# Turning each unit of the Fourier stage by identity products on the four quarters of the TensorE array

## The chip, the cores and the metric

The kernel runs on one core of a Trainium2 chip. The metric is the device time of one execution in microseconds (us). The kernel before was timed three times; the number used is the median. Engines are named as in the profile: PE is TensorE's matmul side, PEld its weight loads, DVE is VectorE, ACT is ScalarE, POOL is GpSimd, SP is SyncE, which here only issues transfers.

## The reference

```python
def reference(x, filt_r, filt_i, moe_w_in, moe_w_out, moe2_w_in, moe2_w_out):
    X = np.fft.rfft(x, axis=1)                     # x: (2, 3008, 256)
    y = np.fft.irfft(X * (filt_r + 1j * filt_i)[None], n=3008, axis=1)
    x = y.reshape(6016, 256).astype(np.float32)
    h = x @ moe_w_in                               # (256, 2048)
    x = np.maximum(0.01 * h, h) @ moe_w_out        # (2048, 256)
    h = x @ moe2_w_in
    r = np.maximum(h, 0.0)
    return (r * r) @ moe2_w_out
```

A filter along the sequence by Fourier transforms, and then two layers of matrix products, everything in float32.

## The kernel before, in words

The sequence length 3008 is 64 times 47, and the transform is done as one over 64 points and one over 47. The channels are worked on in two halves of 128. The first stage is `over_n1` (L906): products of the input with a table over the 64 points, whose results ACT and DVE copy out of PSUM into the tiles TT1A and TT1B, one for each half of the channels, with channels on the 128 partitions. Then come 16 units, eight for each half (UNITS, L15); a unit is four frequencies j (UJ = 4) of both batch rows. The tiles hold for each frequency a real and an imaginary part, each in a stretch of 64 columns of which 48 (R) hold data; the 16 columns between a real and an imaginary part are set to zero at the start (L347, semaphore `n1_pad`).

A unit i goes through these steps, each with its own banks of PSUM:

- `turn(i)` on PE (L922 to L939): eight full transposes, one for each batch row b and frequency k, each of a 128 x 112 piece of TT1 against the 128 x 128 identity `DM[:, 2, :]`. Batch row b goes to PSUM bank b. The last transpose of each batch row increments `s2_ps`.
- `turned(i)` on ACT (L526): two copies, one for each batch row, from bank b into the tile S2 (shown as S in the profile), each started by its own count of `s2_ps`; each increments `s2_sb`. S2 has two buffers.
- `spectrum(i)` on PE (L941): four products with the table TW over the 47 points, each 48 partitions x 64 columns with 512 moving columns (two of them are split in two for the first unit of a half). Real and imaginary rows and the two pairs of frequencies take different quarters of the array. It waits for both copies (`s2_sb` at 2i+2), writes banks 2 and 3 or 4 and 5 in turns, and increments `p_ps`.
- `filtered(i)` on DVE (L748): three operations from PSUM with the filter tile FL (L762, L766 twice), into AF and BF.
- two operations on POOL (L449, L450), which finish the complex product and increment `yf_sb`. Between units POOL also does some of the preparation of the first layer's weights (L351 to L369).
- `inverse(i)` on PE (L960): four products as in `spectrum`, out of AF, into banks 6 and 7. It waits for `yf_sb` and for the copies of the unit before.
- `back(i)` on ACT (L531): two copies from banks 6 and 7 into U.
- `store_u(i)` (L235): SP stores U to the DRAM tensor zu; when a half is complete `load_v` (L251) reads it back in another order as V.

`sequence(c)` (L980) does the last products of the transform out of V, and from L1019 on the two layers run; there each product is a sum of three passes (`passes`, `up`).

The order on PE is written out (L1001 to L1018). After a short start the loop over i issues `spectrum(i+2)`, `turn(i+3)`, `inverse(i)`. The last iterations carry four `sequence` steps of the first half between them (`drained`). The order on ACT (L600 to L614) is `turned(i+3)`, `back(i)`. So the copies of a turn stand between that turn and the next `spectrum` on PE, and `inverse` is what PE has to do meanwhile:

```python
for i in range(UNITS):
    if i + 2 < UNITS:
        spectrum(i + 2)
    if i + 3 < UNITS:
        turn(i + 3)
    if i >= UNITS - 3:
        for c in drained(i):
            sequence(c)
    inverse(i)
```

Ahead of everything PE does eight products of a zero tile WARM (L902) into bank 0.

A float32 product appears in the trace as two MATMUL records and two LDWEIGHTS records, a transpose as one of each.

Of the kernel before, what the change touches and what calls it, by code (L numbers as in the profile page):

```python
# [5 lines left out]
B, S, D, F = 2, 3008, 256, 2048  # L6
# [3 lines left out]
R = 2 * MH  # L10
IM = 64
KR = IM + R
UJ = 4
# [16 lines left out]
def fft_mlp_kernel(nc, x, filt, dft, tab, sgn, w1i, w1o, w2i, w2o, out):  # L30
    f32, f32r = mybir.dt.float32, mybir.dt.float32r
    ALU = mybir.AluOpType
    ACT = mybir.ActivationFunctionType
# [5 lines left out]
    def at(name, shape, dt, offset):  # L39
        return nc.alloc_sbuf_tensor_at(name, shape, dt, offset=base + offset)  # L40
# [13 lines left out]
    S2 = at("S2", [KR, 2, B, UJ, 128], f32, o_wo + 24 * KB)  # L54
    TT1A = at("TT1A", [128, B, 2 * NJ, IM], f32, o_x + 32 * KB)
    TT1B = at("TT1B", [128, B, 2 * NJ, IM], f32, o_x)
    TT1 = [TT1A, TT1B]
    DM = at("DM", [128, 3, 128], f32, o_s + 2 * KB)
# [27 lines left out]
    WARM = at("WARM", [128, 128], f32, o_s)  # L86
# [5 lines left out]
    with ExitStack() as ctx:  # L92
        def sem(name):
            return ctx.enter_context(nc.semaphore(name))

        PS = ctx.enter_context(nc.psum_tensor("PS", [128, 8, 512], f32))
# [11 lines left out]
        s2_ps = sem("s2_ps")  # L108
        s2_sb = sem("s2_sb")
        p_ps = sem("p_ps")  # L110
        n1_pad = sem("n1_pad")
        prod = sem("prod")
        yf_sb = sem("yf_sb")
        u_ps = sem("u_ps")
# [59 lines left out]
        def pair_cols(p):  # L174

            q = p % NP
            return 2 * sum(PAIR_W[:q]), PAIR_W[q]
# [165 lines left out]
        def _(pool):  # L343

            nc.gpsimd.memset(WARM[:, :], 0.0).then_inc(warm_sb, 1)
            for half in range(2):
                nc.gpsimd.memset(TT1[half][:, :, 0::2, R:IM], 0.0).then_inc(n1_pad, 1)  # L347

            WI_STEPS = {k: 4 * n for n, k in enumerate((0, 1, 2, 3, 4, 5, 6, 7))}

# [94 lines left out]
            for i in range(UNITS):  # L445

                a, c = AF[i % RINGS], BF[i % RINGS]
# [35 lines left out]
            for s in range(KU, 2 * NP * KU - KU):  # L483
                p, k, j = s // KU, s % KU, s - KU
# [33 lines left out]
        def _(act):  # L518
# [5 lines left out]
                nc.scalar.activation(rows, ps, ACT.Copy).then_inc(n1_sb[0], 1)  # L524

            def turned(i):  # L526
                for b in range(B):
                    act.wait_ge(s2_ps, 2 * i + b + 1)
                    nc.scalar.activation(S2[:, i % 2, b, :, :].rearrange("p j d -> p (j d)"), PS[0:KR, b, :], ACT.Copy).then_inc(s2_sb, 1)

            def back(i):  # L531

# [62 lines left out]
            def n1_copy_late(c):  # L595
                act.wait_ge(n1_ps[1], c + 1)
                rows, ps = n1_out(c, 1)
                nc.scalar.activation(rows, ps, ACT.Copy).then_inc(n1_late, 1)

            turned(0)  # L600
            turned(1)
            n1_copy_late(CH - 2)
            turned(2)
            n1_copy_late(CH - 1)
            for i in range(UNITS):
# [86 lines left out]
            for s in range(1, SLOTS + 1):  # L692
                p, k = s // KU, s % KU
# [33 lines left out]
            c, w = pair_cols(2 * NP - 1)  # L727
# [171 lines left out]
        @block.tensor  # L899
        def _(pe):  # L900
            pe.wait_ge(warm_sb, 1)
            for _ in range(8):  # L902
                nc.tensor.matmul(PS[:, 0, 0:128], WARM[:, :], WARM[:, :], start=True, stop=True)  # L903
            pe.wait_ge(dft_in, 16)

            def over_n1(c, half):  # L906
# [15 lines left out]
            def turn(i):  # L922

                half, u = i // NU, i % NU
                if i == 0:
                    pe.wait_ge(n1_pad, 2)
                    pe.wait_ge(dft_rest, 16)
                    pe.wait_ge(n1_sb[0], CH)
                if i == NU:
                    pe.wait_ge(n1_sb[1], CH - 2)  # L930
                    pe.wait_ge(n1_late, 2)
                for b in range(B):
                    if i >= 1:
                        pe.wait_ge(s2_sb, 2 * i - 1 + b)
                    for k in range(UJ):
                        q = 2 * (UJ * u + k)
                        mm = nc.tensor.transpose(PS[0:KR, b, 128 * k:128 * k + 128],  # L937
                                                 TT1[half][:, b, q:q + 2, :].rearrange("p q r -> p (q r)")[:, 0:KR], DM[:, 2, :])
                    mm.then_inc(s2_ps, 1)  # L939

            def spectrum(i):  # L941

# [57 lines left out]

            over_n1(CH - LATE, 1)  # L1001
            turn(0)
            over_n1(CH - LATE + 1, 1)
            spectrum(0)
            turn(1)
            over_n1(CH - LATE + 2, 1)
            spectrum(1)
            turn(2)
            over_n1(CH - LATE + 3, 1)
            for i in range(UNITS):  # L1010
# [276 lines left out]
```

## Time and profile before

| | us |
|---|---|
| median of 3 runs | 1069.74 |
| lowest, highest | 1068.79, 1070.24 |
| the profiled execution, its own time | 1068.72 |
| its span in the profile | 1066.7 |
| PE busy | 1059.6 |
| DVE, ACT, POOL busy | 755.7, 564.7, 300.7 |

The span is what the trace covers; the execution's own time is 2.0 us longer than that. Busy time is the time in which at least one instruction of an engine was in progress. Since matmuls are pipelined and their ends are modelled, a group of matmuls shows as busy without a gap even where the array itself pauses for a tenth of a microsecond. The units of the Fourier stage run from 24 us to 78 us of the span; the two layers begin at about 94 us.

### The profile page before, as it was taken

The page shows a single profiled execution, that of the slowest core. Times are in us where ns is not written, and L with a number is a line of the kernel's source. Part 1 is how long each engine was busy: PE and PEld are TensorE (multiplying, and loading weights), DVE is VectorE, ACT ScalarE, POOL GpSimd, SP SyncE. Part 2 cuts the span into 40 slices and gives each one's busy share as a digit, 9 for nine tenths or more (in the row PEclk, how much of TensorE's full clock was granted, in tenths as well). Part 3 has the DMA queues.
Part 4 walks back from the last instruction along what each step waited for, and adds up shares of the span by engine and source line. Part 5 has one row for each costly group of instructions (what it writes and reads, how often), then busy time and mean ns, then how long its engine had stood idle before and what let it go on. Part 6 is the DMA issues. An engine that isn't in the chain of part 4 may idle for free.

```text
span 1066.7 us, 13987 instructions
## 1 busy us (share of the span) xinstructions
PE 1059.6 (99%) x5120; PEld 880.0 (83%) x5120; DVE 755.7 (71%) x1141; ACT 564.7 (53%) x980; POOL 300.7 (28%) x287
## 2 busy tenths in 40 slices
PE   9998999999999999999999999999999999999998
PEld 9558888888888888888999888888888888888998
DVE  2877997767767777676666767667667676676666
ACT  3666554655555555554554544544554554554443
POOL 2997552342342333332220220220220210210000
PEclk9999999999999999999999999999999999999999
DMA  9696000112112112112244000100100100100100
GB/s 321 179 298 224 10 1 1 52 36 61 47 35 68 40 42 67 38 45 57 93 160 163 21 1 1 40 1 1 40 1 1 40 1 1 40 1 1 40 1 35
DMA packets 66724, 61.45 MB, mean 58 GB/s; under 512 B 40688, under 2 KB 53856, under 8 KB 66656
## 3 DMA queue, kind: packets, MB, share of 16 engines
q1 hardware_dynamic: 66160, 60.06, 18.1%
q8 instruction: 41, 0.67, 0.3%
q10 hardware_dynamic: 496, 0.49, 0.1%
q14 instruction: 27, 0.22, 0.1%
HBM read 36.55 MB, written 23.99 MB: 57 GB/s over the span
## 4 chain that ended last, share of the span: by engine, by line
PE 98%; DVE 1%; DMA 1%; ACT 0%; issue 0%; POOL 0%; SPq 0%; DVEq 0%; ACTq 0%; POOLq 0%
PE PS L1021 16%; PE PS L1023 16%; PE PS L1022 16%; PE PS L1029 14%; PE PS L1031 14%; PE PS L1030 14%; PE PS L913 2%; PE PS L937 2%; PE PS L977 1%; PE PS L957 1%; PE PS L997 1%; DMA V<-zu 0%; PE PS L903 0%; DMA zu<-U 0%; DVE YL L792 0%; DVE XL L795 0%
## 5 line engine op out<-in xcount | busy, mean ns | idle before, releaser
L666 ACT ACTIVATE GH<-GF 128x512 fp32r<-128x512 f32 (+1 forms) x384 | 238.7, 622 | 228.0 <-DVE GF L856 116.3
L862 DVE TENSOR_TENSOR GL<-GF,GH 128x512 fp32r<-128x512 f32 (+1 forms) x384 | 260.6, 685 | 105.2 <-ACT GH L666 99.5
L1021 PE MATMUL PS<-GH,WOH 128*128 128x512 f32 (+1 forms) x768 | 296.2, 386 | 0.0
L1022 PE MATMUL PS<-GL,WOH 128*128 128x512 f32 (+1 forms) x768 | 295.8, 385 | 0.0
L1023 PE MATMUL PS<-GH,WOL 128*128 128x512 f32 (+1 forms) x768 | 295.8, 385 | 0.0
L1029 PE MATMUL PS<-XH,WIH 128*128 128x512 f32 (+1 forms) x672 | 259.8, 387 | 2.3 <-DVE XL L795 1.4
L1031 PE MATMUL PS<-XH,WIL 128*128 128x512 f32 (+1 forms) x672 | 258.8, 385 | 0.0
L830 DVE TENSOR_TENSOR GF<-PS,GF 128x512 f32<-128x512 f32 (+1 forms) x96 | 65.3, 680 | 161.7 <-ACT GF L637 161.4
L1021 PEld LDWEIGHTS PS<-GH,WOH 128*128 128x128 f32 x768 | 144.2, 188 | 28.0 <-DVE GL L862 1.5
L1023 PEld LDWEIGHTS PS<-GH,WOL 128*128 128x128 f32 x768 | 144.2, 188 | 26.9
L1022 PEld LDWEIGHTS PS<-GL,WOH 128*128 128x128 f32 x768 | 144.2, 188 | 26.8
L1029 PEld LDWEIGHTS PS<-XH,WIH 128*128 128x128 f32 x672 | 126.2, 188 | 27.1 <-DVE XL L795 1.1
L1030 PE MATMUL PS<-YL,WIH 128*128 128x512 f32 (+1 forms) x384 | 147.8, 385 | 0.0
L1031 PEld LDWEIGHTS PS<-XH,WIL 128*128 128x128 f32 x672 | 126.2, 188 | 23.6
L854 DVE SCALAR_TENSOR_TENSOR GF<-GF 128x512 f32<-128x512 f32 (+1 forms) x192 | 144.0, 789 | 1.6
L637 ACT ACTIVATE GF<-PS 128x512 f32<-128x512 f32 (+1 forms) x96 | 56.6, 589 | 163.7 <-PE PS L1023 163.7
L856 DVE SCALAR_TENSOR_TENSOR GF<-GF 128x512 f32<-128x512 f32 (+1 forms) x192 | 121.6, 674 | 1.7
L1030 PE MATMUL PS<-XL,WIH 128*128 128x512 f32 (+1 forms) x288 | 111.0, 385 | 0.0
L428 POOL TENSOR_TENSOR YL<-YT,XH 128x1024 fp32r<-128x1024 f32 (+1 forms) x22 | 52.6, 2390 | 137.8 <-DVE GL L862 137.8
L660 ACT ACTIVATE GF<-PS 128x512 f32<-128x512 f32 (+1 forms) x96 | 56.7, 591 | 57.5 <-PE PS L1031 57.5
L1030 PEld LDWEIGHTS PS<-YL,WIH 128*128 128x128 f32 x384 | 72.1, 188 | 13.3
L412 POOL TENSOR_TENSOR XT<-YT 128x512 f32<-128x512 f32 (+1 forms) x11 | 14.4, 1308 | 184.3 <-DVE GL L862 184.3
(85 smaller groups left out, 928.2 us busy)
## 6 DMA issues: line engine op xcount, KB each, us to landing
V<-zu SPq DMA_DIRECT2D x12, 512.0 KB, 6.1
zu<-U SPq DMA_DIRECT2D x31, 192.0 KB, 3.6
out_y<-YT SPq DMA_DIRECT2D x5, 1024.0 KB, 4.3
X<-in_x SPq DMA_DIRECT2D x8, 512.0 KB, 8.1
FL<-in_filt SPq DMA_DIRECT2D x16, 224.0 KB, 4.3
wi<-PWH SPq DMA_DIRECT2D x16, 224.0 KB, 2.5
wi<-PWL SPq DMA_DIRECT2D x16, 224.0 KB, 3.1
WIH<-wi SPq DMA_DIRECT2D x8, 448.0 KB, 3.5
```

The source lines that it names most:

```text
L660: nc.scalar.activation(GF[:, g_slot(n), 0:width(s)], PS[:, XB[s % 2], 0:width(s)], ACT.Copy).then_inc(h_sb[UD], 1)
L666: nc.scalar.activation(GH[:, g, 0:width(s)], GF[:, g, 0:width(s)], ACT.Copy).then_inc(g_hi[kind], 1)
L830: nc.vector.tensor_tensor(h, PS[:, YB, 0:w], h, ALU.add).then_inc(h_sb[UA], 1)
L854: nc.vector.scalar_tensor_tensor(h, h, 0.01, h, ALU.mult, ALU.max).then_inc(g_sb[kind], 1)
L856: nc.vector.scalar_tensor_tensor(h, h, 0.0, h, ALU.max, ALU.mult).then_inc(g_sb[kind], 1)
L862: nc.vector.tensor_tensor(GL[:, g, 0:w], GF[:, g, 0:w], GH[:, g, 0:w].bitcast(f32), ALU.subtract).then_inc(g_lo[kind], 1)
L1021: nc.tensor.matmul(acc, wh, xh, start=first, stop=False)
L1022: nc.tensor.matmul(acc, wh, xl, start=False, stop=False)
L1023: return nc.tensor.matmul(acc, wl, xh, start=False, stop=last)
L1029: nc.tensor.matmul(acc, wh, xh, start=first, stop=False, skip_group_check=not first)
L1030: nc.tensor.matmul(acc, wh, lo, start=False, stop=False, skip_group_check=not first)
L1031: return nc.tensor.matmul(acc, wl, xh, start=False, stop=True, skip_group_check=not first)
```

## The change

The eight transposes of a unit become 32 products. Each takes 64 channels (a half h of the 128 partitions), one batch row, one frequency and one part (real or imaginary, 48 columns) of TT1 as its weights, and a 64 x 64 piece of the identity as its moving tile. The half h chooses the rows of the array and the PSUM bank, the part chooses the columns of the array and the PSUM partitions. A bank thus holds one half of the channels for both batch rows. There is one count of four in `s2_ps` for the unit, and one wait ahead of the whole turn in place of one for each batch row. ACT waits for all four before the first of its two copies; its copies are now one for each half of the channels. The zeroing of the columns between the parts falls away with its semaphore, and the products of WARM are spread over banks 0 and 1.

```diff
--- before.py
+++ after.py
@@ -108,7 +108,6 @@
         s2_ps = sem("s2_ps")
         s2_sb = sem("s2_sb")
         p_ps = sem("p_ps")
-        n1_pad = sem("n1_pad")
         prod = sem("prod")
         yf_sb = sem("yf_sb")
         u_ps = sem("u_ps")
@@ -343,8 +342,6 @@
         def _(pool):
 
             nc.gpsimd.memset(WARM[:, :], 0.0).then_inc(warm_sb, 1)
-            for half in range(2):
-                nc.gpsimd.memset(TT1[half][:, :, 0::2, R:IM], 0.0).then_inc(n1_pad, 1)
 
             WI_STEPS = {k: 4 * n for n, k in enumerate((0, 1, 2, 3, 4, 5, 6, 7))}
 
@@ -524,9 +521,10 @@
                 nc.scalar.activation(rows, ps, ACT.Copy).then_inc(n1_sb[0], 1)
 
             def turned(i):
-                for b in range(B):
-                    act.wait_ge(s2_ps, 2 * i + b + 1)
-                    nc.scalar.activation(S2[:, i % 2, b, :, :].rearrange("p j d -> p (j d)"), PS[0:KR, b, :], ACT.Copy).then_inc(s2_sb, 1)
+                act.wait_ge(s2_ps, 4 * i + 4)
+                for h in range(2):
+                    nc.scalar.activation(S2[:, i % 2, :, :, 64 * h:64 * h + 64].rearrange("p b j d -> p (b j) d"),
+                                         PS[0:KR, h, :].rearrange("p (n d) -> p n d", d=64), ACT.Copy).then_inc(s2_sb, 1)
 
             def back(i):
 
@@ -899,8 +897,9 @@
         @block.tensor
         def _(pe):
             pe.wait_ge(warm_sb, 1)
-            for _ in range(8):
-                nc.tensor.matmul(PS[:, 0, 0:128], WARM[:, :], WARM[:, :], start=True, stop=True)
+            for h in range(2):
+                for k in range(UJ):
+                    nc.tensor.matmul(PS[:, h, 128 * k:128 * k + 128], WARM[:, :], WARM[:, :], start=True, stop=True)
             pe.wait_ge(dft_in, 16)
 
             def over_n1(c, half):
@@ -923,20 +922,24 @@
 
                 half, u = i // NU, i % NU
                 if i == 0:
-                    pe.wait_ge(n1_pad, 2)
                     pe.wait_ge(dft_rest, 16)
                     pe.wait_ge(n1_sb[0], CH)
                 if i == NU:
                     pe.wait_ge(n1_sb[1], CH - 2)
                     pe.wait_ge(n1_late, 2)
+                if i >= 1:
+                    pe.wait_ge(s2_sb, 2 * i)
                 for b in range(B):
-                    if i >= 1:
-                        pe.wait_ge(s2_sb, 2 * i - 1 + b)
                     for k in range(UJ):
                         q = 2 * (UJ * u + k)
-                        mm = nc.tensor.transpose(PS[0:KR, b, 128 * k:128 * k + 128],
-                                                 TT1[half][:, b, q:q + 2, :].rearrange("p q r -> p (q r)")[:, 0:KR], DM[:, 2, :])
-                    mm.then_inc(s2_ps, 1)
+                        for h in range(2):
+                            d = slice(64 * h, 64 * h + 64)
+                            c = 64 * (UJ * b + k)
+                            for part in range(2):
+                                mm = nc.tensor.matmul(PS[IM * part:IM * part + R, h, c:c + 64], TT1[half][d, b, q + part, 0:R],
+                                                      DM[d, 2, d], start=True, stop=True)
+                                if b == B - 1 and k == UJ - 1:
+                                    mm.then_inc(s2_ps, 1)
 
             def spectrum(i):
```

## Rows read from the trace of the kernel before

**Rows 1.** The page: span, busy time by engine, granted clock in 40 slices.

```profile
span 1066.7 us, 13987 instructions
PE 1059.6 (99%) x5120; PEld 880.0 (83%) x5120; DVE 755.7 (71%) x1141; ACT 564.7 (53%) x980; POOL 300.7 (28%) x287
...
PEclk9999999999999999999999999999999999999999
```

**Rows 2.** Chain that ended last, in order of time: start, length, what.

```profile
32.66 1.02 PE PS L937 x8
...
52.12 0.86 PE PS L957 x8
52.98 1.01 PE PS L937 x8
53.99 1.02 PE PS L977 x8
...
67.46 1.02 PE PS L937 x8
...
76.83 1.18 PE PS L977 x8
...
78.82 3.54 DMA zu<-U
82.43 3.93 DMA V<-zu
```

**Rows 3.** Nine units: length; busy PE, PEld, DVE, ACT, POOL; clock, DMA share, GB/s.

```profile
39.40:65.50 26.10, 26.10 (x225) 12.52 (x224) 22.80 (x28) 19.53 (x37) 25.32 (x25) 1.00 0.87 256
```

**Rows 4.** Timeline of one unit: start, length, engine, line, what it waited for.

```profile
52.91 1.08 PE L937 MATMUL PS<-DM,TT1B 128*112 128x128 f32 x8
...
53.60 1.09 ACT L529 ACTIVATE S<-PS 112x512 f32<-112x512 f32 x2 [0.24 <-PE PS L937]
...
53.93 1.09 PE L977 MATMUL PS<-AF,TW 48*64 48x512 f32 x8
...
54.73 0.26 PEld L957 LDWEIGHTS PS<-S,TW 48*64 48x64 f32 x8 [0.60 <-ACT S L529]
54.84 1.04 PE L957 MATMUL PS<-S,TW 48*64 48x512 f32 x8
55.16 1.08 ACT L537 ACTIVATE U<-PS 112x512 f32<-112x512 f32 x2 [0.48 <-PE PS L977]
...
55.80 0.32 PE L937 MATMUL PS<-DM,TT1B 128*112 128x128 f32 x1
```

**Rows 5.** Line 957, 30 to 70 us: durations, its waits.

```profile
L957 PE MATMUL PS<-S,TW x108: 589/589/640, 31.6 to 69.8; 48*64 48x512 f32 x108
...
  ACT S L529: 6.4, 12
```

**Rows 6.** PE timeline, the first turns and spectra, four quarters.

```profile
23.81 1.06 PE L937 MATMUL PS<-DM,TT1A 128*112 128x128 f32 x8
...
25.70 0.43 PE L954 MATMUL PS<-S,TW 48*64 48x256 f32 x1
...
25.73 0.64 PE L957 MATMUL PS<-S,TW 48*64 48x512 f32 x1
...
26.73 1.08 PE L937 MATMUL PS<-DM,TT1A 128*112 128x128 f32 x8
...
28.64 1.09 PE L957 MATMUL PS<-S,TW 48*64 48x512 f32 x8
```

**Rows 7.** PE timeline near 84 us; line 997: min/median/max ns and shapes.

```profile
83.65 0.83 PE L997 MATMUL PS<-DM,V 128*128 128x128 f32 x6
...
L997 PE MATMUL PS<-DM,V x192: 222/275/377, 70.3 to 104.2; 128*128 128x128 f32 x184, 128*128 128x64 f32 x8
```

**Rows 8.** ACT copies out of PSUM into a strided output, mean ns.

```profile
L524 ACT ACTIVATE TT1A<-PS 128x512 f32<-128x512 f32 x12 | 7.2, 597 | 14.0 <-PE PS L913 14.0
```

**Rows 9.** POOL timeline at the last unit.

```profile
74.71 1.27 POOL L450 TENSOR_TENSOR AF<-AF,BF 112x512 f32<-112x512 f32 x1
```

## The prediction

> **What bounds the kernel now.** I read the page first. PE is busy for 1059.6 of 1066.7 us at full clock in every slice [rows 1], so time is lost or won where PE's own sequence gets longer or shorter. The change touches only the units of the Fourier stage, so the next view is the chain of waits there. It runs through PE alone: turn, inverse, spectrum, turn, with one turn every 2.90 us ((67.46 - 32.66) / 12) [rows 2]. It leaves PE only behind the last inverse, for the store of U and the read of V, so whatever the units lose comes out at the end one for one, unless something beside them is late first.
>
> Two things lie close below. POOL is busy 25.32 of 26.10 us and DVE 22.80 [rows 3], so a faster PE would soon wait for POOL. And the timeline of a unit [rows 4] shows ACT's part. The turn starts at 52.91. ACT's first copy starts at 53.60, when only half the turn is through, and the pair takes 1.09 to 54.69. The weights of the next spectrum load at 54.73, 0.04 behind, and its products start at 54.84. The weights waited for ACT's copy, here and in nearly every unit (12 times) [rows 5]; the products behind them came only 0.11 later, when the inverse had streamed through. So the copies are hidden behind the inverse with 0.1 us to spare. That slack is the number on which this case turns.
>
> **The change part by part.** I set a turn's start to 0 and follow one unit.
>
> *The switch of the array, removed.* Inverse and spectrum have the same eight records in quarters, but the inverse takes 1.02 in the chain and the spectrum 0.86 [rows 2]. The inverse follows full transposes, the spectrum follows quarters. Part of the 0.16 is weights that are not loaded ahead (640 against 589 ns) [rows 5]. From the spectrum's start to the turn's is 0.96, so 0.1 goes there too [rows 4]. With quarters throughout, each of inverse and spectrum should take 0.86.
>
> *The turn itself, from 8 records to 64.* No row has these products. Six records of 128 columns take 0.83 us, the last of them 0.275, so they start (0.83 - 0.275)/5 = 0.111 apart; a record of 64 columns is 275 - 222 = 53 ns shorter [rows 7], so 0.058. The quarters work side by side: four products start 0.03 us after one another in all [rows 6], and eight records of 512 columns take 0.86 us, not 8 x 0.43 [rows 2]. So 16 records in each quarter take 16 x 0.058 = 0.93 us, against 1.02 now. Bounds: 16 x 0.053 = 0.85 if only the columns count, and 64 x 0.058 = 3.7 if the quarters don't overlap. I take 0.93, since the rows nearest to it (same quarters, same two records for a product) overlap fully. The weights are 48 columns where spectrum has 64, and load ahead.
>
> The trace disagrees with a rule as far as the turn alone goes. A 128-column product costs two records 0.111 apart, a transpose one, so a product in the full array would cost twice the transpose. The Trainium skill, Perfetto Trace Analysis, section Transposes, says to use a transpose for a logical transpose and not a matmul. In the full array that would give a turn of 16 x 0.111 = 1.8 us; four quarters side by side more than repay it.
>
> *ACT's copies, started later.* Now the first starts at 0.69 (53.60 - 52.91), after half the turn. After the change both wait for all four last records. Those start at 15 x 0.058 + 0.02 = 0.89 and last 0.22, until 1.11. From the end of the inverse (53.93 + 1.09 = 55.02) to ACT's copy at 55.16 is 0.14 [rows 4]; that too ends in four quarters with four increments, so I take 0.14 (the bound below is the 0.04 between copy and weights). ACT starts at 1.25. The copies write 64-column pieces with a stride; copies with an output as scattered take 597 ns [rows 8], and two of these, the second begun a tenth of a microsecond ahead of the first one's end, are the 1.09 seen now, so the pair stays at 1.09 and ends at 2.34. The spectrum's weights load at 2.34 + 0.05 = 2.39; today it is 54.73 - 52.91 = 1.82.
>
> *What is queued behind it.* PE has the inverse for the meantime, from 0.93 to 1.79; then it stands still until 2.39, some 0.6 us in every unit. Behind the spectrum stands the next turn, and so the wait comes back in the next round: it is a closed loop, turn, copies, spectrum, turn. The spectrum now takes 0.05 for its weights and 0.86. The loop is 2.39 + 0.91 = 3.30 us, against 2.90. ACT's copies of U fit (they wait behind S's until 2.3 and end by 3.4, and the next inverse starts at 4.2). DVE and POOL, with 2.5 and 2.8 us a unit [rows 3], are no longer close. The moved wait of the turn, both copies instead of one, costs nothing: the spectrum just ahead of it has waited for the same count.
>
> *Edits at nothing.* Zeroing and its semaphore: POOL does it while the inputs load. WARM over two banks: the same eight products.
>
> **The sum.** In the start-up a turn and a spectrum have a block of first-stage products between them. The first spectrum comes 1.89 behind the first turn (25.70 - 23.81) [rows 6]; that becomes 2.39, so +0.50. The next two go from 1.91 (28.64 - 26.73) [rows 6] to 2.39, +0.48 each, and behind each of the three spectra the lost switch gives back 0.11. Turn 3 is late by 0.50 + 0.48 + 0.48 - 0.33 = 1.1. From turn 3 to turn 15 there are twelve rounds of 0.40: +4.8. Between the last turn and the last spectrum, +0.4. Behind that the order has PE's sequence steps and full products as before. POOL ends its last operation at 74.71 + 1.27 = 75.98 [rows 9], 0.85 ahead of the last inverse at 76.83 [rows 2], and both move together. Sum +6.3 us, against the profiled execution's own 1068.72: 1075.0. The median of the runs lies 1.0 above that execution, so 1069.74 + 6.3 = 1076.0.
>
> Bounds of this forecast: increments seen at once (-0.1 a unit) and columns alone (-0.08) take 0.18 x 16 = 2.9 off, 1073. A turn of 1.1 us (+0.17 a unit) adds 2.7, 1079.
>
> **The rivals.**
>
> *Issue bounds the turn.* No stretch of the trace asks PE for 64 small records in a row. In a burst that was queued beforehand they start about 10 ns apart [rows 6], but a queue that has to be refilled may be slower. The bounds are 0.010 and 0.058 a record. Half way in ratio is 0.024, so a turn of 64 x 0.024 = 1.55 us, 0.62 more than I take, and 16 times that on top: 1086. Against it: the spectrum's wait lasts 0.6 us, in which the queue can fill.
>
> The Trainium skill, TensorE: Matmul & The Clock Gate, section Back-to-back issue gap, gives a floor of about 25 ns from start to start however small the product. By that figure (an estimate from the page) the turn would take 1.6 us and the kernel 1087. The 10 ns starts contradict it for different quarters, which is why this rival has only 0.14.
>
> *No overlap at all.* Small products with their own weights keep the quarters apart: 3.7 us a turn, 2.8 more, 1076 + 45 = 1121. Against it stand rows 2 and 6. 0.03.
>
> *The clock.* PE pauses 0.6 us in each unit, which it doesn't now, and the granted clock, full throughout [rows 1], could fall to its lower level (1.2 GHz) in the stage. All of PE's work there would double, some 1.8 us a unit: about 1105. 0.03.
>
> *Faster.* The wait doesn't arise, because ACT starts earlier or its copies overlap more than 1.09 us for the pair says. Then PE is bound by its own 0.86 + 0.93 + 0.86 = 2.65 us, and soon by POOL, 2.80 a unit [rows 3], so 0.1 in each of thirteen units, and up to 1.0 in the start-up, where POOL has spare time: 2.3 us less, 1067.4. It decides where the copies end before the inverse does, 1.79 behind the turn's start; I have 2.34, so 0.55 would have to go. 0.08, mostly for what I misread in the loop.
>
> *No effect.* The switch's gain and the wait cancel, 1069.7. That needs the copies at 1.9 and is an accident: 0.02.
>
> **How the numbers follow.** Forecast 0.70, issue 0.14, no overlap 0.03, clock 0.03, faster 0.08, none 0.02. The range starts at the forecast's lower end with a microsecond of allowance, 1072, and reaches over the issue rival, 1087. Outside are about 0.17. A measurement of this kernel tells about 0.2%, 2.1 us, from no change: slower 0.90; faster 0.06 (1067.4 is just past that bound, so part of its 0.08 goes to same); same 0.04.
>
> **What would show it.** In the profile after: turns 3.3 us apart in the chain, with pieces of ACT's S copies (L525 to L528) in it where it was PE alone; the spectrum's weights idle for ACT in every unit, and PE itself now idle with them; a turn of 64 records in about 0.93 + 0.2 us from first start to last end; the inverse at 0.86 in place of 1.02; PE's busy share in the units near 80%; DVE idling longer for PE in front of L762. The stage after the units should keep its length. The forecast is wrong if the turns come under 2.9 us apart, if ACT's S copies begin less than 0.9 us after a turn's start, or if the turn takes more than 1.2 us.

## The result and the profile after

The changed kernel takes 1075.38 us (median of 4 runs, 1074.98 to 1075.83) against 1069.45, now the median of 4 runs too. The ratio is 1.0056, with a 95% interval of 1.0044 to 1.0068. The forecast was 1076.0. The profiled execution's span is 1073.0 us, 6.3 longer than before, for a forecast of +6.3. One execution of one kernel below (1173.7 us, of the one with the turns further ahead) fell in a slower state of the chip and is left out of that kernel's median.

The first lines of the page after, with the clock in 40 slices and the instruction queue:

```profile
span 1073.0 us, 15777 instructions
...
PE 1060.6 (99%) x6016; PEld 882.5 (82%) x6016; DVE 757.2 (71%) x1141; ACT 562.8 (52%) x980; POOL 298.3 (28%) x285
...
PEclk9999999999999999999999999999999999999999
...
q8 instruction: 48, 0.79, 0.3%
```

PE's busy time grew by 1.0 us only, the span by 6.3. The clock stayed full. PE doesn't do more; it stands. Where it stands is in the chain (start, length, what):

```profile
34.12 1.02 PE PS L939 x64
...
56.99 1.02 PE PS L939 x64
58.05 0.47 issue
58.52 0.60 ACT S L526
59.16 1.09 PE PS L960 x8
...
73.32 1.02 PE PS L939 x64
...
83.06 1.18 PE PS L980 x8
...
85.05 3.74 DMA zu<-U
```

In [rows 2] the chain of a unit was turn, inverse, spectrum, all PE. Now the inverse (L980) is gone from it in all units but one, and ACT's copies (L526) stand between the turn (L939) and the spectrum (L960). Turns come (73.32 - 34.12)/12 = 3.27 us apart, against 2.90. The last inverse starts at 83.06 where it started at 76.83, 6.2 later, and what follows keeps its length to 0.1 us.

The timeline of a unit after, for [rows 4]:

```profile
56.81 1.07 PE L939 MATMUL PS<-DM,TT1B 64*48 64x64 f32 x64
...
57.70 1.04 PE L980 MATMUL PS<-AF,TW 48*64 48x512 f32 x8
...
58.03 1.08 ACT L526 ACTIVATE S<-PS 112x512 f32<-112x512 f32 x2 [1.21 <-PE PS L939]
...
59.16 0.21 PEld L960 LDWEIGHTS PS<-S,TW 48*64 48x64 f32 x8 [1.30 <-ACT S L526]
59.16 1.09 PE L960 MATMUL PS<-S,TW 48*64 48x512 f32 x8 [0.42 <-ACT S L526]
...
60.07 1.08 PE L939 MATMUL PS<-DM,TT1B 64*48 64x64 f32 x64
```

From the turn's start: the inverse at 0.89, ACT's copy at 1.22, the spectrum's weights at 2.35, and from there 0.91 to the next turn. Before, ACT began at 0.69 and the spectrum's weights loaded at 1.82. In [rows 4] the spectrum's products came 0.11 behind their weights, held by the inverse; here both start together, held by ACT alone. The bracket on the PE line shows 0.42 idle. That is less than the array stood: the inverse's products start at 57.70, and two records of 0.43 in each quarter keep it until 58.56, so it stood 0.60 before 59.16. The ends of the records are modelled, and the bracket counts from the modelled end.

### The profile page after: what moved, and what is told of

Its sections match the earlier page's. It is cut to its first block, busy times and chain, and to the rows that moved or that the text cites. A ratio compares the mean times of both kernels' runs of the same rounds, so it can differ in the third digit from the quotient of the medians.

```text
span 1073.0 us, 15777 instructions
## 1 busy us (share of the span) xinstructions
PE 1060.6 (99%) x6016; PEld 882.5 (82%) x6016; DVE 757.2 (71%) x1141; ACT 562.8 (52%) x980; POOL 298.3 (28%) x285
## 4 chain that ended last, share of the span: by engine, by line
PE 96%; ACT 1%; DVE 1%; DMA 1%; issue 1%; POOL 0%; SPq 0%; DVEq 0%; ACTq 0%; POOLq 0%
PE PS L1024 16%; PE PS L1025 16%; PE PS L1026 16%; PE PS L1032 14%; PE PS L1033 14%; PE PS L1034 14%; PE PS L912 2%; PE PS L939 2%; PE PS L960 2%; ACT S L526 1%; PE PS L1000 1%; PE PS L980 0%; DMA V<-zu 0%; PE PS L902 0%; DMA zu<-U 0%
```

## The experiments

The theory: the loss is a closed loop of turn, ACT's two copies and spectrum, closed by having both copies wait for the whole turn. The first rival: the 64 small records of a turn are the cost. The second: PE's own work is the bound and the pauses are an effect of how ends are drawn.

**The wait alone, in the kernel before.**

```diff
 def turned(i):
+    act.wait_ge(s2_ps, 2 * i + 2)
     for b in range(B):
-        act.wait_ge(s2_ps, 2 * i + b + 1)
         nc.scalar.activation(S2[:, i % 2, b, :, :]..., PS[0:KR, b, :], ACT.Copy).then_inc(s2_sb, 1)
```

> Full transposes as before; only ACT's two copies both wait for the whole turn. Theory (closed loop turn, copies, spectrum): ACT's first copy starts 1.1 us after the turn's start in place of 0.69, the weights of the spectrum load at 1.12 + 1.09 + 0.04 = 2.25, the spectrum takes 0.05 + 0.86 and the switch of the array 0.1, so turns come 3.27 us apart, and the kernel takes about 1075.4 us: the whole loss comes from the wait. Rival (the 64 small products of a turn make the loss, the wait is hidden): turns 2.90 apart, 1069.5 us.

Measured: 1075.2 us, ratio 1.0049 (1.0032 to 1.0066). Its timeline:

```profile
57.05 1.09 PE L937 MATMUL PS<-DM,TT1B 128*112 128x128 f32 x8
...
58.17 1.09 ACT L529 ACTIVATE S<-PS 112x512 f32<-112x512 f32 x2 [1.07 <-PE PS L937]
...
59.30 0.21 PEld L957 LDWEIGHTS PS<-S,TW 48*64 48x64 f32 x8 [1.04 <-ACT S L529]
...
60.33 0.43 PE L937 MATMUL PS<-DM,TT1B 128*112 128x128 f32 x2
```

ACT at 1.12, weights at 2.25, next turn at 3.28, each as expected. One moved wait costs the kernel with the full transposes all that the change cost. So in this loop the quarter products are worth nothing. From the spectrum's weights to the next turn they give back 0.12 us (0.91 in place of 60.33 - 59.30 = 1.03), and they lose 0.10 again because ACT sees the end of the turn later (1.22 in place of 1.12).

**More work for PE in its pause.** The products of the inverse's second half are issued twice.

```diff
                             mm = nc.tensor.matmul(o, TW[rows, 2 + part, :], y, start=True, stop=True)
+                            if js == 1:
+                                mm = nc.tensor.matmul(o, TW[rows, 2 + part, :], y, start=True, stop=True)
                         mm.then_inc(u_ps, 1)
```

> The changed kernel with the two products of the inverse's second half issued twice, 0.43 us of PE work more in each unit, with the same results. Theory: PE pauses 0.6 us behind each inverse, so the work falls into the pause: 1075.4, at most 1 us more. Rival (PE's own work is the bound, the pauses are an effect of the modelled ends): 16 x 0.43 = 6.9 more, 1082.

Measured: 1079.29 us, ratio 1.009 (1.0075 to 1.0105), 3.9 above the changed kernel. It is neither number. The chain shows why:

```profile
56.34 0.86 PE PS L980 x6
57.20 0.86 PE PS L982 x4
...
59.82 0.86 PE PS L980 x6
```

The expectation mis-sized the edit. Both doubled products lie in two quarters of the array, which now have four records of 512 columns each where the other two have two: the step is 1.72 us in those quarters, 0.86 more, not 0.43. A unit became 59.82 - 56.34 = 3.48, 0.21 longer. So 0.65 of 0.86 fell into the pause, near the 0.60 of the timeline. Without a pause 16 x 0.86 = 13.8 us would have come. The second rival is out.

**Each turn twice, in both kernels.** In the changed kernel all 32 products are issued twice; in the kernel before the eight transposes.

```diff
-                for b in range(B):
+                for b, last in ((0, False), (1, False), (0, True), (1, True)):
...
-                                if b == B - 1 and k == UJ - 1:
+                                if last and b == B - 1 and k == UJ - 1:
```

```diff
-                    for k in range(UJ):
+                    for k in (*range(UJ), *range(UJ)):
                         q = 2 * (UJ * u + k)
                         mm = nc.tensor.transpose(...)
```

> The changed kernel, each turn's 32 products issued twice over. Theory: a turn lies wholly in the closed loop, so each unit becomes longer by 16 records a quarter, 0.86 to 0.93 us, turns 4.15 apart, 1075.4 + 16 x 0.88 = 1089.5 us. If a turn were partly hidden: less. If issue bound it (25 ns a record): 1.6 us a unit more, 1101.

> The kernel before with each batch row's four full transposes issued twice: 8 records and 0.87 us of PE work more in a unit, with few instructions. Theory: PE bounds every unit there, 1069.5 + 16 x 0.87 = 1083.4 us, and nothing on top, since 16 more instructions a unit are no strain on PE's supply. The doubled quarter turn brought 27 us where its stream explains 14; if a like excess comes here, it was not the count of instructions.

Measured: 1102.6 us for the quarters (ratio 1.0311, 1.0293 to 1.033), 27.2 above the changed kernel; 1083.06 for the transposes (ratio 1.0124), as expected to 0.4 us. The two differ in what a doubled turn asks of PE: 64 more product records a unit or 8. The PE timeline of the quarters:

```profile
48.88 1.97 PE L939 MATMUL PS<-DM,TT1A 64*48 64x64 f32 x128
...
53.04 1.97 PE L939 MATMUL PS<-DM,TT1A 64*48 64x64 f32 x128
...
58.68 1.49 PE L939 MATMUL PS<-DM,TT1A 64*48 64x64 f32 x90 [0.76 <-issue]
...
71.61 0.31 PE L939 MATMUL PS<-DM,TT1B 64*48 64x64 f32 x2 [1.80 <-issue]
...
74.85 3.64 PE L939 MATMUL PS<-DM,TT1B 64*48 64x64 f32 x128
```

and its busy time by stretch (length; busy PE, PEld, DVE, ACT, POOL; clock, DMA share, GB/s):

```profile
38.00:43.00 5.00, 4.99 (x146) 4.03 (x148) 2.54 (x3) 0.89 (x2) 2.36 (x3) 0.66 0.02 3
69.80:73.10 3.30, 1.32 (x12) 0.34 (x12) 0.97 (x2) 1.14 (x3) 2.25 (x2) 0.93 0.12 42
73.10:79.50 6.40, 6.40 (x144) 4.17 (x144) 2.54 (x3) 1.86 (x4) 2.70 (x5) 0.51 0.49 141
```

Three things stand in these rows. Where nothing disturbs it, a unit is 53.04 - 48.88 = 4.16 us, as expected: 0.89 more for 16 more records in each quarter, 56 ns a record. Those make 14 of the 27 us. Then there are gaps in the middle of a turn, with 'issue' as the releaser (0.76, 1.80): PE waited for nothing that the profile names. The trace has eight of them of 0.18 us and more, 6.5 us in all. And after the longest of them the granted clock was 0.51, its lower level of 1.2 GHz, over 6.4 us, where a turn took 3.64 in place of 1.97. PE had done 1.32 us of work in the 3.3 before it. The Trainium skill, TensorE: Matmul & The Clock Gate, section Part 1: The HAM clock gate, has two fixed levels of the clock, the lower one behind idle time; the row agrees. The clock had fallen once before, behind a gap of 1.25 us at 35.27 and a wait for ACT: the mean from 38 to 43 us is 0.66. The two stretches cost some 5 us (half of 6.4, and 0.34 x 5 = 1.7). With 14 and 6.5 that is nearly the 27.

**The turn ahead of the spectrum, in both kernels.**

```diff
-                if i + 2 < UNITS:
-                    spectrum(i + 2)
                 if i + 3 < UNITS:
                     turn(i + 3)
+                if i + 2 < UNITS:
+                    spectrum(i + 2)
```

> The changed kernel, with the turn of unit i+3 issued ahead of the spectrum of unit i+2 in the loop. Theory: turn and spectrum of neighbouring units no longer stand in one loop with the copies; between two turns PE has 0.86 + 0.86 + 0.86 = 2.6 us of work and the copies need 2.4, so POOL (2.8 us a unit) bounds the stage: turns about 2.8 apart in the middle, 1068 us (1066.5 to 1070). Rival (the quarter products or their issue slow the stage whatever stands around them): stays at 1075.

> The kernel before with the same exchange of turn and spectrum. Theory: it is bound by PE's own 2.89 us a unit, which the exchange doesn't change: turns 2.9 apart, 1069.5 us (up to 1070.5, since POOL gets its work a spectrum later). Rival (the exchange is good for anything of its own): under 1068.

Measured: 1073.68 us for the changed kernel (ratio 1.0039, 1.0024 to 1.0054), only 1.7 less; 1070.47 for the kernel before (1.0007, 0.9998 to 1.0017), within the expectation. The chain of the first:

```profile
37.59 0.67 DVE BF L764
...
38.33 1.28 POOL AF L446
39.61 1.25 POOL AF L447
...
40.91 1.09 PE PS L980 x8
...
44.37 0.86 PE PS L980 x8
45.23 0.90 PE PS L939 x64
46.13 0.86 PE PS L960 x8
```

Turn, spectrum and inverse do follow one another at 0.90, 0.86, 0.86, so the loop is open and the small records stream well for a while. But the exchange puts each spectrum one turn later and so DVE, POOL and then the inverse, on which PE now waits: a new loop, which the expectation left out. 'Issue' gaps of 0.28, 0.75 and 0.40 us come on top.

**The turns one unit further ahead.**

```diff
+                if i == 0:
+                    turn(3)
                 if i + 2 < UNITS:
                     spectrum(i + 2)
-                if i + 3 < UNITS:
-                    turn(i + 3)
+                if i + 4 < UNITS:
+                    turn(i + 4)
```

with ACT's copies in the same order, in the changed kernel, in the kernel before, and in the changed kernel with three of POOL's weight operations moved behind the last unit.

> The changed kernel with the turns one unit further ahead: in the loop spectrum(i+2), turn(i+4), inverse(i), ACT's copies likewise. This opens the loop of turn, copies and spectrum without moving the spectrum behind the turn, which in the last trace put DVE, POOL and the inverse into a new loop. PE's own work is 0.86 + 0.85 + 0.86 = 2.6 us a unit, turn to turn over the copies 2.4, POOL 2.8 with its weight work. Theory: turns 2.8 apart, 1068 us (1066.5 to 1069.5). Rival (64 small records of a turn disturb their neighbours in any order): 1072 or more.

> The kernel before with the same order as the last one. Theory: PE's 2.89 us a unit bound it, turns 2.9 apart, 1069.5 us, no change. So what the last kernel gains over this one is what the quarters and the missing switches are worth where nothing waits. Rival (the gain is the order's own): this one gains as much as the last.

> As e8, and POOL's three pieces of the second weight block (2.4 us in all) are moved from between the units to behind the last one. If POOL bounds the stage in e8, its end comes up to 2.4 us earlier: 1066 us (1065 to 1068). Rival (PE or DVE is the bound there): the same time as e8.

Measured: 1073.7 us (ratio 1.004, 1.0026 to 1.0054), 1069.42 (1.0002, 0.9993 to 1.0011), 1073.2 (1.0035, 1.0023 to 1.0048). The second is as expected, the first missed by 6 and the third by 7. No trace of the first is read here. The chain of the third:

```profile
41.92 0.89 PE PS L940 x61
...
42.83 0.86 PE PS L981 x7
43.69 0.85 PE PS L961 x7
44.54 0.89 PE PS L940 x61
...
52.39 0.70 issue
...
56.88 1.28 POOL AF L446
...
78.83 4.65 POOL WIL L366 x6
...
91.48 0.42 POOL WIF L360
```

and of the kernel before with the turns ahead:

```profile
50.80 1.02 PE PS L939 x8
51.83 1.02 PE PS L979 x8
52.85 0.86 PE PS L959 x8
53.70 1.02 PE PS L939 x8
```

A unit is 44.54 - 41.92 = 2.62 us with the quarters and 53.70 - 50.80 = 2.90 with the full transposes. That is the change's own worth where nothing waits: 0.28 us a unit, as the forecast had it for PE (2.65). Two things take it away. From 56.88 on this chain runs through POOL. The units' part of POOL's work ends at 78.83, 2.9 us later than before [rows 9], although 2.4 us of its work had been moved. The third spectrum had started at 34.96 in place of 31.57, since at the start each turn with its copies still precedes its spectrum, and POOL, which the chain doesn't leave from 56.88 on, can't make that up. Behind the units the chain stays on POOL's weight pieces, the moved ones among them, until 91.9. So what was moved out of the units came back in front of the layers. And PE again has a gap that only 'issue' explains (0.70 at 52.39; in the kernel with the turn ahead of the spectrum the same product of the same spectrum starts at 53.39, behind 0.75).

**Mixed.** Units 0 to 4 turned as before, the rest by quarters and one unit further ahead.

```diff
+        WHOLE = 5
...
+                if i < WHOLE:
+                    ... (turn and copies as in the kernel before)
+                    return
...
-                if i + 3 < UNITS:
+                if i + 3 < WHOLE:
                     turn(i + 3)
+                elif i + 4 < UNITS:
+                    turn(i + 4)
...
                 inverse(i)
+                if i + 4 == WHOLE:
+                    turn(WHOLE)
```

> Units 0 to 4 turned by full transposes with a wait for each batch row and in the old order, so that the spectra come 2.9 us apart while DVE and POOL get going; units 5 to 15 by quarter products, their turns one unit further ahead. Theory: turn 5 costs spectrum 4 one turn (0.9 us) once, from there turns come 2.6 to 2.8 apart in place of 2.9, ten times; PE's pauses at the ends of its instruction blocks (about 1 us each where nothing covers them, seen in the last traces) take part of it back: 1068.5 us (1067 to 1070). Rival (the order itself is what cost 4 us in the last runs): 1072 or more.

> As the mixed kernel, with POOL's three pieces of the second weight block behind the last unit: if POOL bounds the mixed kernel, 1 to 2 us less than it (1067); if PE or its instruction supply does, the same time, or more since the pieces now stand in front of the next blocks.

Measured: 1071.52 us (12 runs from 1069.81 to 1075.0; ratio 1.0017, 1.0008 to 1.0025) and 1074.45 (ratio 1.0038, 1.0026 to 1.005). The first misses its range by 1.5 us. Of its chain:

```profile
38.22 1.08 ACT U L544 x2
39.30 0.98 ACT S L535 x2
...
40.33 1.11 PE PS L962 x64
...
46.66 1.20 issue
...
57.09 1.25 issue
...
63.41 1.28 POOL AF L450
```

The last inverse starts at 80.19, 3.4 us later than before. Three things hold it. Where the order changes, PE waits for ACT, whose copies of turn 5 stand behind its copies of U, and spectrum 5 starts at 42.12 in place of 40.31; 0.5 of these 1.8 us was there from the start. Two gaps of 1.2 us follow. From 63.41 to 71.71 the chain is POOL's. With POOL's pieces moved, the last inverse of the second kernel starts at 78.25, 1.9 us earlier, so POOL did hold the end of the units, as its expectation had it. But in that trace the store of U behind it takes 6.22 us in place of 3.85, and nothing is won; why it does, no run tells. No version that was run beats the kernel before.

## Why the prediction was right

- **What bounds the kernel.** Right: PE, with ACT's copies 0.1 us below. The wait alone (1075.2) shows that this slack decided.
- **The turn.** Forecast 0.93 us, the last record starting at 0.89 and ending at 1.11. The turn's records span 1.07 to 1.08 us, the last of them starting at 0.86, and the inverse's products start at 0.89. Quarters overlap fully; 56 ns a record from the doubled turn, for 58.
- **The switch.** Right: the spectrum to the next turn takes 0.91 (forecast 0.05 + 0.86), inverse and spectrum 0.86 each where nothing waits.
- **ACT's start.** Forecast 1.25, measured 1.22; the pair 1.08, as before, with its new output; the spectrum's weights at 2.35, forecast 2.39.
- **The round.** 3.27, forecast 3.30. Over twelve rounds this is 4.4 us, forecast 4.8.
- **Start-up and tail.** Turn 3 is 1.46 us late in the chain (34.12 against 32.66), forecast 1.1; some 0.24 of it was there at the first turn (24.17 against 23.93) and varies between kernels that share all code up to it. From turn 15 to the last inverse 9.74 us against 9.37, +0.37, forecast +0.4. The two misses, -0.4 and +0.4, cancel. That the sum comes out to a tenth is luck in part; the mechanism and the size of the round are not.
- **The rival of issue.** It costs nothing in this kernel, because the pause hides it, as the text argued. But it is real where PE is asked for more in the same time: the doubled turn and the opened orders with quarter products whose traces are read here had such gaps. Its form was wrong, though. It is no steady 24 ns a record, since undisturbed records take 56 ns in a quarter and four quarters run at once. It comes as single gaps of up to 1.8 us. The floor of about 25 ns from start to start that the Trainium skill gives (TensorE: Matmul & The Clock Gate, section Back-to-back issue gap) shows in no turn here: 128 records in 1.75 us (1.97 less the last one's 0.22) are 14 ns.
- **The clock.** It stayed full with PE pausing 0.6 us in 3.27. Of the traces only that of the doubled turn has it lower, in the two stretches shown. But some untraced executions of the opened and mixed orders have a mean clock of 0.997 or 0.998 over the whole kernel, among them the slowest (1075.0 us at 0.997 for the mixed one, whose nine at full clock lie between 1069.81 and 1072.24). So a part of what those orders missed may be the clock's.
- **What was said of the profile.** PE's busy share near 80% was wrong: PE is busy 35.15 of the 40 us from 36 to 76, 88%. The array's own 2.65 of 3.30 us would be 80%, but the modelled ends cover part of each pause.

What the gaps are, the traces tell. The instruction queue moves 41 packets of 16 KB before, 48 after and 56 with the doubled turn. PE's own instructions, with its weight loads and semaphore waits, are 10473, 12265 and 14313: 1792 more for 7 packets, 2048 more for 8, so one packet for 256 of PE's instructions. If PE's instructions are counted in the order of their starts, the one behind a gap is number 705, 1217, 1473, 1729, 1985, 2497, 2753, 3009, 3265, 4289, 4801 or 5057. Each is 193 more than a multiple of 256, and this holds for all 17 gaps of 0.1 us and more in the first 110 us of the traces in which the whole of PE stands with 'issue' as the releaser. They lie in five kernels, all with quarter products: the doubled turn, the turn ahead of the spectrum, the third of the turned-ahead kernels and both mixed ones. PE starts again 1.2 to 1.6 us behind the end of a packet. In the kernel before, the packet ends 11 us and more ahead of each such place in the units. In the changed kernel, from its third such place on, it is 1.2 to 3.8 us, and at number 2497 (the inverse at 64.70, the one unit whose chain still runs through the inverse) 1.39; the pause covers it. So a gap is PE waiting for its next block of instructions, by its place in the program and by its time; no run changed the supply alone. Packets start from 0.2 to over 3 us after PE has begun the block before, and what sets that is open.

Left untried: ACT's copies by batch row with the quarter products, which would open the loop in place. The two row halves of the array write two banks, so a copy of one batch row would read a bank that PE still writes for the other, and all eight banks are in use.

## What to carry to other kernels

Before making a step on the busiest engine cheaper, look at how its result is handed on: a step that is consumed in two halves hides its own length, and one that signals at its end puts the whole of it, and the consumer's whole time, into the loop. A weight load that already waits for ACT with 0.1 us to spare tells this before the change is made. And count instructions: 112 more a unit were free behind a wait, and cost up to 1.25 us at a time in the orders that took the wait away.

## What the runs showed of the hardware

Products on different quarters overtake one another across steps. In the changed kernel with the turns further ahead and POOL's pieces moved, records of a turn start after the first records of the inverse that the program has behind it:

```profile
54.72 0.61 PE L981 MATMUL PS<-AF,TW 48*64 48x512 f32 x2
...
54.79 0.27 PE L940 MATMUL PS<-DM,TT1B 64*48 64x64 f32 x2
```

PE's instructions come in blocks of 256, and in stretches with some 60 and more instructions a microsecond (162 in 2.62 us, 290 in 4.16) PE at times waits for the next block, up to 1.8 us; with 162 in 3.27 us the wait stayed hidden. The longest such gap, 1.80 us, was followed by 6.4 us at a granted clock of 0.51, at which the same work took some 3 us longer.
